# One fp32 matmul for the steady attention units, with the probabilities' copy moved on ScalarE

## The reference

```python
for c in range(24):                       # chunks of 32 queries
    k_full = concat(mem_k, k[c*32-16 : c*32+40])      # 8 memory positions and the window
    v_full = concat(mem_v, v[c*32-16 : c*32+40])
    scores = q_c @ k_full.T / 8
    a = exp(scores - max(scores)); a = a / (sum(a) + 1e-9)
    out_c = a @ v_full
x = out as [3072, 512]
h = x @ w_in;  g = s * relu(h)**2 + b;        x = g @ w_out      # w_in 512 x 2048
h = x @ w_in2; g = h * sigmoid(1.702 * h);    out = g @ w_out2
```

## Time and profile before

| what | value |
|---|---|
| median of 3 runs | 1192.25 us (1191.92 to 1192.62) |
| the profiled execution | 1191.04 us, of which the span is 1189.2 us |
| TensorE busy | 1170.7 us, 98% |
| VectorE busy | 895.9 us, 75% |
| ScalarE busy | 698.6 us, 59% |
| GpSimd busy | 401.2 us, 34% |
| granted TensorE clock, mean of the span | 1.00 of 2.4 GHz |
| DMA | 104.28 MB, 88 GB/s |

### The profile page before, as it was taken

One profiled execution on the slowest core, in us unless ns is written; L12 is line 12 of the kernel. 1 busy time (PEld: TensorE's weight loads), 2 busy tenths in 40 slices (PEclk: granted clock), 3 DMA queues, 4 the chain that ended last, 5 costly groups with the idle time before them and its releaser, 6 DMA issues.

```text
span 1189.2 us, 19643 instructions
## 1 busy us (share of the span) xinstructions
PE 1170.7 (98%) x6170; PEld 1010.4 (85%) x6170; DVE 895.9 (75%) x2261; ACT 698.6 (59%) x1907; POOL 401.2 (34%) x412
## 2 busy tenths in 40 slices
PE   8999999999999999999999999999999999999998
PEld 5899999999888888888888888888888888888887
DVE  7787777777777777667888957889577888577663
ACT  7788767767776776444445744446444456444452
POOL 3865222222222222323563124640245521244200
PEclk9999999999999999999999999999999999999999
DMA  7753322313132232113422424224234224222231
GB/s 149 170 136 87 66 52 52 76 43 64 35 76 63 56 89 60 37 36 104 142 71 79 146 91 142 71 72 142 71 107 142 71 80 150 89 71 71 71 115 62
DMA packets 167691, 104.28 MB, mean 88 GB/s; under 512 B 99495, under 2 KB 144039, under 8 KB 167591
## 3 DMA queue, kind: packets, MB, share of 16 engines
q1 hardware_dynamic: 166368, 102.82, 31.4%
q10 hardware_dynamic: 1223, 0.23, 0.1%
HBM read 89.26 MB, written 13.76 MB: 87 GB/s over the span
## 4 chain that ended last, share of the span: by engine, by line
PE 85%; ACT 6%; DVE 4%; issue 3%; POOL 1%; DVEq 0%; ACTq 0%; POOLq 0%
PE psum L976 25%; PE psum L933 22%; PE psum L935 18%; PE psum L908 11%; PE psum L851 2%; PE psum L875 2%; DVE arena L1430 2%; ACT arena_raw L1101 2%; PE psum L862 2%; ACT arena L1088 2%; ACT arena L1096 1%; PE psum L839 1%; DVE arena L1454 1%; PE psum L838 1%; PE psum L773 1%
## 5 line engine op out<-in xcount | busy, mean ns | idle before, releaser
L976 PE MATMUL psum<-weights 128*128 128x512 f32 (+1 forms) x1344 | 337.6, 386 | 0.0
L976 PEld LDWEIGHTS psum<-weights 128*128 128x128 f32 x1344 | 252.2, 188 | 49.2
L935 PE MATMUL psum<-g_hi,weights 128*128 128x384 f32 (+1 forms) x768 | 223.2, 362 | 0.0
L908 PE MATMUL psum<-arena,weights 128*128 128x384 f32 (+1 forms) x960 | 215.9, 360 | 0.2 <-DVE ffn L1490 0.2
L908 PEld LDWEIGHTS psum<-arena,weights 128*128 128x128 f32 x960 | 166.4, 188 | 9.1 <-DVE ffn L1490 0.4
L1533 DVE TENSOR_TENSOR arena_raw<-psum,arena_raw 128x512 f32<-128x512 f32 (+1 forms) x160 | 109.0, 681 | 85.5 <-PE psum L976 83.8
L712 POOL TENSOR_TENSOR arena_raw<-arena_raw,small 96x256 f32<-96x256 f32 x96 | 58.6, 610 | 271.7 <-DVE small L1450 261.3
L935 PEld LDWEIGHTS psum<-g_hi,weights 128*128 128x128 f32 x768 | 139.5, 188 | 8.8
L935 PE MATMUL psum<-g_lo,weights 128*128 128x384 f32 (+1 forms) x384 | 138.1, 360 | 0.0
L1430 DVE TENSOR_TENSOR arena<-psum,arena 128x96 fp32r<-128x96 f32 x336 | 83.2, 275 | 68.3 <-ACT arena L1096 65.9
L1101 ACT ACTIVATE arena_raw<-arena_raw,small 96x128 f32<-96x128 f32 x224 | 88.0, 394 | 78.0 <-DVE small L1439 77.6
(11 more groups left out here) (132 smaller groups left out, 2201.1 us busy)
## 6 DMA issues: line engine op xcount, KB each, us to landing
arena_raw<-in_moe_w_out_dram SPq DMA_DIRECT2D x128, 256.0 KB, 4.0
arena_raw<-in_moe_w_in_dram SPq DMA_DIRECT2D x64, 256.0 KB, 3.0
arena_raw<-in_k_dram SPq DMA_DIRECT2D x31, 240.0 KB
arena_raw<-in_v_dram SPq DMA_DIRECT2D x30, 240.0 KB
arena_raw<-x_scratch SPq DMA_DIRECT2D x3, 2048.0 KB, 10.0
arena_raw<-in_q_dram SPq DMA_DIRECT2D x31, 192.0 KB
out_dram<-result SPq DMA_DIRECT2D x5, 1024.0 KB, 5.1
result<-in_moe_w_in_dram SPq DMA_DIRECT2D x16, 256.0 KB, 3.8
```

The source lines that it names most:

```text
L908: last = nc.tensor.matmul(dst, w[:, kt * P:(kt + 1) * P], x, start=(kt + i == 0), stop=(kt == KT - 1 and i == 2))
L935: last = nc.tensor.matmul(acc[c][:, 0:n], w[:, piece], g, start=start, stop=stop)
L976: last = nc.tensor.matmul(bank_of[bank][:, 0:width(i)], w[:, k * P:(k + 1) * P], x[:, k, :], start=(k + t == 0), stop=(k == 1 and t == 2))
```

## The change

The steady units multiply probabilities by v with one matmul on fp32 operands. The transposed probabilities have one fp32 buffer (two slots) in place of a high and a low part, and ScalarE's copy into it stands in kind 2, ahead of `copy_x_hi`, and waits for `qk_ready` of n+3 in place of `qk_transposed`. v is loaded by DMA straight into one of two slots; GpSimd no longer splits it, and SyncE waits for the last `attend` of the block that had the slot. `mask_and_max` signals once per head, and `exp` waits for its head.

```diff
@@ -208,10 +208,8 @@
         attn = raw_area(ATTN, 6 * DM)
         qk_hi = area(ATTN + 3072, 704).rearrange("p (a c) -> p a c", a=2)
         qk_lo = area(ATTN + 3776, 704).rearrange("p (a c) -> p a c", a=2)
-        pT_hi = area(ATTN + 4480, 384).rearrange("p (a c) -> p a c", a=2)
-        pT_lo = area(ATTN + 4864, 384).rearrange("p (a c) -> p a c", a=2)
-        v_hi = area(ATTN + 5248, 1024).rearrange("p (a c) -> p a c", a=2)
-        v_lo = area(ATTN + 6272, 1024).rearrange("p (a c) -> p a c", a=2)
+        pT = raw_area(ATTN + 4480, 384).rearrange("p (a c) -> p a c", a=2)
+        v_steady = raw_area(ATTN + 5248, 1024).rearrange("p (a c) -> p a c", a=2)
 
 
         def x2_parts(i, t):
@@ -497,12 +492,10 @@
                 load_qk(j, slice(0, H), qk_loaded[j % 2])
 
             def load_steady_v(j):
-                if HP * (j - 1) < FIRST:
-
-                    sp.wait_ge(s_attended, 2 * ((FIRST // HP - 1) // 2 * 2 + 1))
-                else:
-                    sp.wait_ge(v_ready, nth(HP * j - 1) // HP)
-                load_v(j, v_raw, v_loaded)
+
+                if HP * (j - 2) >= FIRST:
+                    sp.wait_ge(attended, nth(HP * (j - 1) - 1))
+                load_v(j, v_steady[:, j % 2, :], v_loaded[j % 2])
 
             def load_w_in(f):
 
@@ -697,16 +690,6 @@
                                         s_inv[:, i % 2, :].unsqueeze(2).to_broadcast([QT, 4, P]), ALU.mult
                                         ).then_inc(s_probs_ready, 1)
 
-            def split_v(j):
-                i = j - FIRST // HP
-                pool.wait_ge(v_loaded, 32 * (i + 1))
-                if i >= 2:
-                    pool.wait_ge(attended, nth(HP * (j - 1) - 1))
-                nc.gpsimd.tensor_copy(v_hi[:, j % 2, :], v_raw).then_inc(v_hi_done, 1)
-                pool.wait_ge(v_hi_done, i + 1)
-                nc.gpsimd.tensor_tensor(v_lo[:, j % 2, :], v_raw, v_hi[:, j % 2, :].bitcast(F32), ALU.subtract
-                                        ).then_inc(v_ready, 1)
-
             def normalize(n):
                 pool.wait_ge(inv_ready, nth(n))
                 nc.gpsimd.tensor_tensor(probs[:, n % 2, :, :], probs[:, n % 2, :, :],
@@ -735,11 +717,8 @@
                         split_w_out(f + CAST)
                     for pos in range(24 * (NF * mm + f), 24 * (NF * mm + f + 1)):
                         for kind, n in AT.get(pos, ()):
-                            j = n // HP + 1
                             if kind == 1 and there(n + 2) and pool_normalizes(n + 2):
                                 normalize(n + 2)
-                            if kind == 1 and n % HP == 1 and there(HP * j) and j > FIRST // HP:
-                                split_v(j)
                     if mm == M0 - 1:
                         if f == LAST_STEPS + 1:
                             sum_x2(0)
@@ -844,7 +823,7 @@
                     pe.wait_ge(zeros_ready, 1)
                     pe.wait_ge(s_max_ready, 4 * HALVES)
                 if there(n - 1):
-                    pe.wait_ge(max_ready, nth(n - 1))
+                    pe.wait_ge(max_ready, 2 * nth(n - 1))
                 if there(n - LEAD):
                     pe.wait_ge(x_ready, nth(n - LEAD))
                 for i, (a, c) in enumerate(((qk_hi, qk_hi), (qk_hi, qk_lo), (qk_lo, qk_hi))):
@@ -867,14 +846,12 @@
                 if there(n - 1):
                     pe.wait_ge(x_ready, nth(n - 1))
                 if there(n + LEAD - 2):
-                    pe.wait_ge(max_ready, nth(n + LEAD - 2))
+                    pe.wait_ge(max_ready, 2 * nth(n + LEAD - 2))
                 if hp == 0:
-                    pe.wait_ge(v_ready, j - FIRST // HP + 1)
+                    pe.wait_ge(v_loaded[j % 2], 32 * ((j - FIRST // HP) // 2 + 1))
                 pe.wait_ge(pT_ready, nth(n))
-                for i, (a, c) in enumerate(((v_hi, pT_hi), (v_hi, pT_lo), (v_lo, pT_hi))):
-                    last = nc.tensor.matmul(bank_o, a[:, j % 2, hp * P:(hp + 1) * P], c[:, n % 2, :],
-                                            start=(i == 0), stop=(i == 2))
-                last.then_inc(attended, 1)
+                nc.tensor.matmul(bank_o, v_steady[:, j % 2, hp * P:(hp + 1) * P], pT[:, n % 2, :], start=True, stop=True
+                                 ).then_inc(attended, 1)
 
             def group(kind, n):
                 if kind == 1:
@@ -1088,16 +1065,9 @@
                     last = nc.scalar.activation(qk_hi[parts, n % 2, cols], bank_qk[parts, source], ACT.Copy)
                 last.then_inc(qk_hi_done, 1)
 
-            def split_pT_hi(n):
-
-                if there(n + LEAD - 1):
-                    act.wait_ge(qk_transposed, nth(n + LEAD - 1))
-                act.wait_ge(probs_transposed, nth(n))
-                nc.scalar.activation(pT_hi[:, n % 2, :], bank_pT, ACT.Copy).then_inc(pT_hi_done, 1)
-
             def exp(n):
-                act.wait_ge(max_ready, nth(n))
                 for h in range(2):
+                    act.wait_ge(max_ready, 2 * nth(n) - 1 + h)
                     nc.scalar.activation(probs[:, n % 2, h, :], probs[:, n % 2, h, :], ACT.Exp, scale=-1.0,
                                          bias=exp_bias[:, n % 2, h:h + 1], accum_out=total[:, n % 2, h:h + 1]
                                          ).then_inc(exp_done, 1)
@@ -1108,6 +1078,13 @@
                     last = nc.scalar.activation(probs[:, n % 2, h, :], probs[:, n % 2, h, :], ACT.Copy,
                                                 scale=inv_total[:, n % 2, h:h + 1])
                 last.then_inc(probs_ready, 1)
+
+            def copy_pT(n):
+
+                if there(n + LEAD - 1):
+                    act.wait_ge(qk_ready, nth(n + LEAD - 1))
+                act.wait_ge(probs_transposed, nth(n))
+                nc.scalar.activation(pT[:, n % 2, :], bank_pT, ACT.Copy).then_inc(pT_ready, 1)
 
             def copy_x_hi(n):
                 if there(n + LEAD - 1):
@@ -1135,9 +1112,9 @@
                         exp(n + 2)
                     if there(n + LEAD) and there(n):
                         split_qk_hi(n + LEAD)
+                else:
                     if there(n + 1):
-                        split_pT_hi(n + 1)
-                else:
+                        copy_pT(n + 1)
                     if there(n):
                         copy_x_hi(n)
                     if there(n + 2) and not pool_normalizes(n + 2):
@@ -1424,8 +1401,6 @@
 
             def split_qk_lo(n):
                 dve.wait_ge(qk_hi_done, nth(n))
-                if there(n - LEAD + 1):
-                    dve.wait_ge(pT_hi_done, nth(n - LEAD + 1))
                 for (parts, cols), source in QK_PIECES:
                     last = nc.vector.tensor_tensor(qk_lo[parts, n % 2, cols], bank_qk[parts, source],
                                                    qk_hi[parts, n % 2, cols].bitcast(F32), ALU.subtract)
@@ -1436,10 +1411,10 @@
                 if there(n - LEAD + 1):
                     dve.wait_ge(x_hi_done, nth(n - LEAD + 1))
                 for h in range(2):
-                    last = nc.vector.tensor_tensor_reduce(
+                    nc.vector.tensor_tensor_reduce(
                         out=probs[:, n % 2, h, :], in0=bank_s[0:QT, h * P:(h + 1) * P], in1=masks[:, mask_of(n // HP), :],
-                        scale=-SCALE, scalar=-MASKED, op0=ALU.add, op1=ALU.min, accum_out=exp_bias[:, n % 2, h:h + 1])
-                last.then_inc(max_ready, 1)
+                        scale=-SCALE, scalar=-MASKED, op0=ALU.add, op1=ALU.min, accum_out=exp_bias[:, n % 2, h:h + 1]
+                        ).then_inc(max_ready, 1)
 
             def invert(n):
                 dve.wait_ge(exp_done, 2 * nth(n))
@@ -1448,11 +1423,6 @@
                 if there(n - 2):
                     dve.wait_ge(probs_ready, nth(n - 2))
                 nc.vector.reciprocal(inv_total[:, n % 2, :], total_e).then_inc(inv_ready, 1)
-
-            def split_pT_lo(n):
-                dve.wait_ge(pT_hi_done, nth(n))
-                nc.vector.tensor_tensor(pT_lo[:, n % 2, :], bank_pT, pT_hi[:, n % 2, :].bitcast(F32), ALU.subtract
-                                        ).then_inc(pT_ready, 1)
 
             def split_x_lo(n):
                 dve.wait_ge(x_hi_done, nth(n))
@@ -1474,8 +1444,6 @@
                         invert(n + 2)
                     if there(n + LEAD) and there(n):
                         split_qk_lo(n + LEAD)
-                    if there(n + 1):
-                        split_pT_lo(n + 1)
                 else:
                     if there(n + LEAD - 1):
                         mask_and_max(n + LEAD - 1)
```

6 lines of the change are left out of this document (1 added, 5 removed).

## The result

The changed kernel takes 1176.19 us (median of 4 runs, 1175.73 to 1177.56) against 1192.37 for the kernel before (4 runs on the same chip, 1191.92 to 1192.62): ratio 0.9867, 95% interval 0.985 to 0.9884, so 16 us less and not 10. Its profiled execution took 1176.61 us, span 1174.8; in profiled spans the gain is 14.4, because the profiled execution of the kernel before was 1.3 us under the median of its runs and that of the changed kernel 0.4 over.

What follows compares the result with a forecast made beforehand. TensorE was taken as the bound, standing still about 19 us, mostly before the probability transposes. 11 saved later plus 1 in the first stage, less 2 paid at attend, gave -10 us: profile 1181.0, median 1182.2, range 1177 to 1190.

Steps and rivals of the forecast that it cites:

- The later stages: Stages after the first: of 14 us of TensorE stalls, 2 stay at 480 columns, 1 at stage changes; 11 saved.
- the mean turn of ScalarE and VectorE: Exp to exp, 3.5 and 4.2 alternating, average 3.85 against TensorE's 3.67 at 480 columns; becomes 3.4 to 3.6.
- POOL isn't on the chain, so nothing is counted: GpSimd's split of v: removing 28 casts and 28 subtractions counted as no gain; shorter VectorE instructions left in the lower end.
- One matmul for three: attend on TensorE: one fp32 matmul at 0.33 replaces three at 0.31, +2 us over 112 units, between +1 and +13.
- B: Rival: every attend pays a stopped engine's fp32 start, 0.43 for 0.31; 13.4 paid, 12 saved: 1193.7; chance 0.07.
- rival C: TensorE's array passes alone set attend's time, 0.33 for 0.25 by skill pages; +9 paid, 12 saved: 1189.3; chance 0.05.
- The test that the prediction named: TensorE's step from start of attend to start of score: 0.33 expected, 0.43 under B; over 0.4 means wrong.
- the new waits: ScalarE's pT copy waits for VectorE's q and k low parts, some 0.9 where nothing lies between; mask_and_max waits for copy_x_hi.
- A: Rival: the pT copy's new place is the next wait; half or more of stalls stay, 1186 to 1190.5; chance 0.19.
- D: Rival: pT comes as late as before, so TensorE's probability transposes still wait; 0 to 3 saved, 1191 to 1194; chance 0.07.
- The first stage: ScalarE the busier engine: up to 5 us of new waits against 8 less; +1 us saved, between 4 lost and 4 saved.
- just enough: 0, bound 1 us: SyncE's queue, first stage: w_out load behind a slipped v load keeps 3.8 us for its transfer; cost 0, bound 1 us.

Runs made afterwards that it cites:

- e7: Kernel before with only the maximum signalled per head: 1182.93 us, ratio 0.9918.
- e13: e14 with the maximum signalled per head, pT difference still on VectorE: 1182.94 us, ratio 0.9917.
- e3: Changed kernel with ScalarE's pT copy back in the first group of the unit, right after the q and k high parts: 1173.93 us, ratio 0.985.
- e12: e14 without the pT difference, still one signal for both maxima: 1175.89 us, ratio 0.986.
- e14: Kernel before with only one fp32 matmul in attend, v in slots and no GpSimd split; pT difference kept, its result unused: 1189.21 us, ratio 0.9971.
- e8: Changed kernel with the matmul of attend issued twice into the same bank: 1209.74 us, ratio 1.0142.
- e1: Changed kernel with the maximum signalled once for both heads: 1178.82 us, ratio 0.989.

## Why the prediction was too small

**The bound and the stalls** were read rightly: 19 us of TensorE stopped, 5 in the first stage and 14 later. Counted one by one they are 5.0 and 13.5, with 1.1 more ahead of `attend`, and 0.025 at each of 44 restarts in the stages with 384 and 480 columns (the first transpose steps 0.110 after a stop, 0.086 in the stream): 15.7 later and not 14.

**The later stages are the term that failed**: "gone but for 2 at the stage with 480 columns, where 3.6 is close to 3.67, and 1 at stage changes: 11 saved". Measured is 14.4 + 96 x 0.011 for the dearer `attend` = 15.5. Of the 4.5 missed, 2.0 are the stalls held back for the 480-column stage, where none was left (1.0 at the stage changes is right); 1.7 are the stalls undercounted; 0.8 is not accounted for. The 2 held back come from a wrong mechanism. The prediction judged that stage by the mean turn of ScalarE and VectorE against TensorE's unit, with the 3.50 read from an exp that had itself waited behind the rectifier. The signal per head should have brought the mean turn under 3.67; in e7 it stayed at 3.82, in e13 at 3.85, with stops of 0.34 in every second unit. What ended last in every second unit was a path from TensorE's product over ScalarE's rectifier, exp and copy and VectorE's low parts back to the transposes, with `split_pT_lo` (0.36) as its last link; without that link the stop of 0.34 is gone in e3 and, but for one unit, under 0.1 in e12. The direction came out right because the same instruction stands in both accounts, and that is luck as far as the mechanism goes. At 384 columns the runs fit the turn over the maximum: the signal alone takes 5.1 us of stops to 0.7 (e7), and no stopped unit was followed back there. No run moved the rectifier's place, which would test the other end of the path.

**GpSimd**: "POOL isn't on the chain, so nothing is counted" was a step that failed too. With the fp32 `attend` paid, e14 is 3.5 us faster than before, so v without GpSimd's split is worth 4.7 us by the ratios, 3.4 by the spans, with the parts in that order. By stops it is 1.1 before `attend` and 1.3 before the transposes of the 384-column stage; the rest is not resolved. An engine off the chain lengthened an instruction of one that was on it, and the group's mean of 681 ns at 384 columns (120 to 300 us), where `gate` took 613, would have shown it. These stops were among the stalls that the prediction gave to the turn, so they are not a gain on top of the 15.5.

**One matmul for three**: +2 predicted, 112 x 0.011 = 1.2 measured (0.323 for 0.312; e8's second matmul took 0.322). B falls. Of rival C one half holds: the Trainium skill, "FP8 and Floating Point Precision", TensorE Precision Notes, has four passes for true fp32. The estimate from that, 4 x 192 columns at 2.4 GHz = 0.32 us, agrees with e8's 0.322. The 82.5 ns for each of the three do not hold, they took 104: the Trainium skill, "TensorE: Matmul & The Clock Gate", Back-to-back issue gap, gives that formula for an isolated gap and says that it counts too little for small matmuls in a stream with weight loads, which rival C left out. The test that the prediction named, start of `attend` to start of `score`, reads 0.19 (133.92 to 134.11 above) and is no measure, since the matmul before it stepped 0.32: the next record begins early behind a two-record matmul. Doubling the instruction was.

**The pT copy**: the new waits appeared as named and cost TensorE nothing in the later stages (A and D fall). The gain came from the part that the change removes, not from where it put the copy (e3).

**The maximum per head**: counted in the turn and so never priced. Alone it is worth 9.7 us (e7), after the other parts 1.2 (e12 to e3) to 2.7 (e1), which whole runs can't tell from nothing and the stage with 480 columns shows as 1.1 and 1.6.

**The first stage**: +1 predicted, between 4 lost and 4 saved; measured -0.57, of which 0.2 is the dearer `attend`. The w_out load behind the v load, "just enough: 0, bound 1 us", was not enough: 1.79 us of ScalarE's wait at one unit and a stop of 1.7 behind it. By parts: one matmul and v in slots +0.6, no pT difference -1.1, signal per head -1.0, the copy's new place +2.0. The prediction weighed up to 5 us of new waits against 8 us freed; by these parts it was 2.0 against 2.1.

Together: predicted profile 1181.0, measured 1176.6; later stages +4.5, `attend` +0.8, first stage -1.4, the rest 0.5 outside these stages. By the ratios the change is one matmul and v in slots -3.5, no pT difference -13.2, signal per head -1.2, copy moved +2.0: -15.9 us. The two middle parts depend on their order: with the signal first it gives -6.4 and the pT difference -8.0.

## What to carry to other kernels

Don't test a stall against a mean turn of two engines: take one stopped unit and follow it back, instruction by instruction, until it reaches the bound engine again, and see whether the removed instruction is on that path. Engines that wait for one another all show the same mean turn, so an agreement of means names no cause. Two edits that shorten the same path don't add up, so price each with and without the other. Compare an instruction's longest time with its median before calling another engine free: work off the chain, here GpSimd's, may be lengthening it.
